# Opening of a two-layer feed-forward kernel: main channels rounded first, and three small steps given to GpSimd

## The reference, cut to what matters

```python
# x: 2 x 4096 x 192, weight: 8 heads x 7 taps
w = softmax(weight, axis=-1)                  # exp(w - max) / (sum + 1e-9)
out[b, s, h, :] = sum_k w[h, k] * x_pad[b, s + k, h, :]   # causal mix of 7 tokens
x = out.reshape(8192, 192)
h = x @ w_in_1                                # 192 x 2048
x = (h * sigmoid(h)) @ w_out_1                # 2048 x 192
h = x @ w_in_2
g = where(h > 0, h, exp(min(h, 0)) - 1)
return g @ w_out_2                            # 8192 x 192, float32
```

## Time and profile before

| what | value |
|---|---|
| runs | 1066.47 to 1066.49 us, median 1066.49 |
| the profiled execution | 1067.03 us |
| its span, first to last instruction | 1065.3 us |
| TensorE busy | 1060.8 us (100%) |
| VectorE, ScalarE, GpSimd busy | 772.0, 638.9, 15.5 us |
| granted TensorE clock, mean | 1.00 |
| chain that ended last | TensorE 100% |

### The profile page before, as it was taken

The page is one execution under the profiler, slowest core; times in us unless marked ns, Lnnn a source line. Parts: engine busy times, 40 slices in busy tenths (PEclk is TensorE's granted clock), DMA queues, the critical chain, the costliest instruction groups (busy, mean ns, idle before and its releaser), DMA issues.

```text
span 1065.3 us, 22927 instructions
## 1 busy us (share of the span) xinstructions
PE 1060.8 (100%) x9728; PEld 1054.7 (99%) x9728; DVE 772.0 (72%) x932; ACT 638.9 (60%) x753; POOL 15.5 (1%) x23
## 2 busy tenths in 40 slices
PE   9999999999999999999999999999999999999998
PEld 8999999999999999999999999999999999999998
DVE  7866679888856647988876654898887664488777
ACT  8767765545566756454666566645465666564544
POOL 2300000000000000000000000000000000000000
PEclk9999999999999999999999999999999999999999
DMA  6510100001000000000110000000011000000001
GB/s 195 104 33 16 54 1 1 17 16 31 16 17 16 17 1 2 11 6 16 31 31 1 17 17 1 1 16 11 7 31 31 2 1 1 1 1 17 12 5 31
DMA packets 19571, 22.28 MB, mean 21 GB/s; under 512 B 3088, under 2 KB 14352, under 8 KB 19472
## 3 DMA queue, kind: packets, MB, share of 16 engines
q1 hardware_dynamic: 16992, 19.64, 6.5%
q0 software_dynamic: 2176, 0.79, 0.7%
q10 hardware_dynamic: 304, 0.40, 0.1%
HBM read 14.52 MB, written 6.29 MB: 20 GB/s over the span
## 4 chain that ended last, share of the span: by engine, by line
PE 100%; ACT 0%; issue 0%; DVE 0%
PE acc L867 51%; PE hid L847 47%; PE acc L998 1%; PE acc L1005 0%; PE acc L976 0%; PE acc L847 0%; PE acc L964 0%; PE acc L967 0%; PE acc L966 0%; ACT stg L442 0%; DVE zero L541 0%
## 5 line engine op out<-in xcount | busy, mean ns | idle before, releaser
L847 PE MATMUL hid<-x,wi 64*128 64x512 f32 x4335 | 658.9, 376 | 0.0
L847 PEld LDWEIGHTS hid<-x,wi 64*128 64x128 f32 x4335 | 545.8, 186 | 1.4 <-DVE wi L591 0.4
L867 PE MATMUL acc<-ghi,wo 64*128 64x512 f32 x3036 | 518.0, 376 | 0.0
L867 PE MATMUL acc<-glo,wo 64*128 64x512 f32 x2024 | 409.1, 376 | 0.0
L867 PEld LDWEIGHTS acc<-ghi,wo 64*128 64x128 f32 x3036 | 406.3, 186 | 0.7 <-issue 0.4
L660 DVE TENSOR_TENSOR glo<-g,ghi 128x1024 fp32r<-128x1024 f32 x214 | 261.3, 1221 | 188.8 <-ACT g L508 136.7
L508 ACT ACTIVATE g<-hid 128x1024 f32<-128x1024 f32 x213 | 217.3, 1020 | 163.8 <-PE hid L847 163.8
L867 PEld LDWEIGHTS acc<-glo,wo 64*128 64x128 f32 x2024 | 292.1, 186 | 0.6 <-DVE glo L649 0.4
L492 ACT ACTIVATE ghi<-hid 128x1024 fp32r<-128x1024 f32 x125 | 128.0, 1024 | 168.2 <-PE hid L847 168.1
L668 DVE SCALAR_TENSOR_TENSOR g<-hid,g 128x1024 f32<-128x1024 f32 x87 | 106.6, 1225 | 3.0
L666 DVE TENSOR_SCALAR g<-g 128x1024 f32<-128x1024 f32 x87 | 60.4, 694 | 60.6 <-ACT g L508 60.4
(11 more groups left out here) (90 smaller groups left out, 370.3 us busy)
## 6 DMA issues: line engine op xcount, KB each, us to landing
stg<-w_in SPq DMA_DIRECT2D x16, 256.0 KB, 3.4
outT<-stg SPq DMA_DIRECT2D x16, 256.0 KB, 2.0
xa<-x_rows SPq DMA_DIRECT2D x15, 259.0 KB, 3.1
stg<-w_out SPq DMA_DIRECT2D x16, 192.0 KB, 4.1
outT<-tail SPq DMA_DIRECT2D x16, 128.0 KB, 2.3
xb<-x_rows SPq DMA_DIRECT2D x30, 65.5 KB, 2.9
wo<-w_out POOLq DMA_DIRECT2D x4, 128.0 KB, 4.8
xa<-x_rows ACTq DMA_DIRECT2D x1, 259.0 KB, 3.0
```

Of the source, the lines that this page charges most:

```text
L847: return eng.matmul(hidden_part(u, t), wt, in_turn(mv), start=t == home and n == 0, stop=t == home and n == 4 if u < LAG else t != home an ...
L867: return eng.matmul(acc[s % 2][:, bank, :], wt[rows, 2 * j + t, cols], in_turn(mv), start=leads and j == 0 and n == 0, stop=not leads and ...
```

## The change

GpSimd gets three steps at the head of its list: it makes part 0 of the rounded last channels of chunk 0, rounds the output weights of piece 0, and makes the two low rests of piece 2, which leaves VectorE's list. ScalarE rounds the main channels ahead of its copy of `mix0`, makes parts 1 to 3 alone after a wait for part 0, and no longer rounds the output weights of piece 0. Waits are added so that counting semaphores stay in order.

```diff
-    APART = (4, 5, 6, 7)
+    APART = (2, 4, 5, 6, 7)
...
@@ gpsimd @@
+            eng.wait_ge(s_tap, 4)
+            eng.wait_ge(s_tapb, NTAP)
+            eng.tensor_scalar(rest_hi(0, 0, LOW)[:, 0:HT], mixb[LOW, :], tstat[LOW, 5:6], None, ALU.mult)\
+               .then_inc(s_chib, 1)
+            eng.wait_ge(s_chib, 1)
+            eng.wait_ge(s_stgo[0], 16)
+            eng.tensor_copy(wo[0][:, 0:2, 0:D], stg_out(0)).then_inc(s_woh, 1)
+            eng.wait_ge(s_woh, 1)
+            eng.wait_ge(s_xlo, 3)
+            low_in_rest(2)
             low_in_rest(4)
...
@@ scalar, hi_out @@
                 eng.wait_ge(s_stgo[q % NSTG], 16 * (q // NSTG + 1))
+                if q == 1:
+                    eng.wait_ge(s_woh, 1)
                 eng.activation(wt[:, :, 0:D], stg_out(q), ACT.Copy).then_inc(s_woh, 1)
...
@@ scalar @@
             hi_in(0)
             hi_in(1)
+            eng.wait_ge(s_tap, 4)
+            conv_hi_a(0)
             eng.wait_ge(s_mix0, 1)
             eng.activation(mixb[:, :], mix0, ACT.Copy).then_inc(s_tapb, NTAP)
-            eng.wait_ge(s_tap, 4)
-            conv_hi_a(0)
             hi_in(2)
-            for part in range(4):
+
+            eng.wait_ge(s_chib, 1)
+            for part in range(1, 4):
                 conv_hi_b(0, part)
             eng.wait_ge(s_tab, 2)
             eng.activation(tstat[:, 6:7], tstat[:, 7:8], ACT.Silu).then_inc(s_tab, 1)
-            hi_out(0)
...
@@ vector @@
             low_in_rest(0)
             low_in_main(2)
-            for q in range(1, 3):
-                low_in_rest(q)
+            low_in_rest(1)
             low_out(0)
```

## The result

The changed kernel takes 1067.91 us (median of 20 runs, 1067.72 to 1068.45), the kernel before 1066.49 (20 runs, 1066.45 to 1066.94): ratio 1.0013, 95% interval 1.0007 to 1.0019. It is 1.42 us slower. That is clear of the interval, though less than the 0.2% which I called the least that counts, and it lies outside my range (1066.2 to 1067.0).

The account below looks back on a forecast made before the run. TensorE, 100% busy, was taken as the bound, with ScalarE setting its waits at 26.5 and 30.7 us. Start 0.00, main channels 0.00, first gate -0.06, late low weights 0.00 gave -0.06: 1066.43 us by the median, range 1066.2 to 1067.0.

Parts of the forecast that it names:

- The start: First real matmul stays at 10.60 us, set by the array's own 0.31 us switch from full to half height; gain 0.00.
- second rival: ScalarE, not the array, sets TensorE's real start: about 10.50, 0.10 us more gained, 1066.3 us; 8%.
- Step 1: ScalarE rounds main channels before copying mixb: worth nothing, since the array is ready later; mixb's copy ends 10.12 instead of 9.84.
- Step 2: GpSimd makes part 0 of the last channels in 0.45 us (0.29 to 0.90), working from 10.61 to about 10.96; hidden.
- the sign that the forecast fails: The forecast fails as a whole if a one-input operation of GpSimd takes over 1 us.
- Step 3: ScalarE makes three parts of the last channels instead of four, ending at 12.60 us; TensorE needs all four at 13.07.
- The first rival: GpSimd is late and TensorE stalls at 13.07 us: up to +1.26 less 0.06, 1067.7 us; 32%.
- TensorE's pair of 13.07: The matmul pair at 13.07 us that needs all four parts of the last channels; forecast to start without a gap.
- Step 4: GpSimd rounds one piece of output weights in 0.6 us; saves 0.06 on ScalarE, leaves 0.03 us to spare at TensorE.
- Step 5: GpSimd makes piece 2's low rests by 14.3 us; first gate's wait shrinks up to 0.2, taken back at 26.5.
- From page to median: Forecast 1066.97 us against the profiled 1067.03, then 1066.43 for the median, that execution being 0.54 above it.

Follow-up runs that it names:

- f4_before_one_more: The kernel before with VectorE's memset of the zeros cut in two, so every later VectorE instruction stands one place further on; 1067.05 us.
- e1_part0_scalar: The changed kernel, but ScalarE makes part 0 again; GpSimd keeps the output-weight rounding and the low rests of piece 2; 1067.05 us.
- h2_weights_alone: The kernel before with only GpSimd rounding the output weights of piece 0; 1066.68 us.
- e2_part0_alone: The kernel before with part 0 alone given to GpSimd, ScalarE waiting for it; 1066.59 us.
- g3_changed_two_more: The changed kernel with VectorE's memset of the zeros cut in three and nothing else; 1067.60 us.

## Why the prediction was wrong

**The start**: the gap between full-height and half-height matmuls was read rightly, the time at which it falls wrongly. The last warm-up matmul starts at 9.62 + 0.82 - 0.38 = 10.06 and the first half-height one at 10.37, 0.31 again:

```profile
9.62 0.82 PE L1013 MATMUL acc<-zero 128*128 128x512 f32 x3
10.37 0.48 PE L862 MATMUL hid<-x,wi 64*128 64x512 f32 x2
```

But 10.60 was that of one execution. In others the warm-up ends earlier, and then the main channels (VectorE's share of them ends at 9.93 to 9.98) set the start, as in the traces that start at 10.03 to 10.08. This is the second rival's mechanism, at 8%, though not its time. Step 1, which gave the new order nothing and a delay of 0.28 for mixb without a price, was wrong for them: TensorE then asks for the last channels 0.5 earlier too, and the new order costs 0.27 alone and 0.78 together with part 0.

**Step 2, part 0, is the step that failed first**, in both its terms. The price was taken from an operation without an operand in memory to scale by, and my upper end from a two-input one: 0.45, at most 0.90. It measured 0.92 free of all company, about 0.72 of it once it has its turn, and 1.69 in its place, over the 1 us that I had named as the sign that the forecast fails. By the best-case figure of the Trainium skill (GPSIMD Engine Reference, on performance against the Vector engine) the estimate was 0.38, less than half; for the plain rounding of 384 elements, 0.50 measured, the estimate of 0.58 by that page is not exceeded. And the turn: I gave it to GpSimd by order of arrival, from one meeting where VectorE's next operation came 0.6 us later. Here L592 came 0.23 later and went first, 0.75 more.

**Step 3** (the fourth part at 12.60) fell with it: 13.58. **The first rival** was the right mechanism, at the right place: TensorE's pair of 13.07, due at 12.85 after the earlier start, came at 13.69, 0.84 late, and 0.10 for the restart. I gave it 32% and up to 1.26 us; its measured 0.95 lies within.

**Step 4**: the rounding at 0.50 for 0.6 was sized well. Its 0.06 on ScalarE didn't show: L518 starts at 15.29, 0.2 after ScalarE's last idle began, for it waits for TensorE as said.

**Step 5**: the first gate's wait shrank by 0.21, as forecast. That what lies behind 26 us would only shift with ScalarE was wrong. I read two turns of GpSimd and VectorE, and passed over the idle of 0.41 "issue" in VectorE's row at 26.08, which decides who goes first. Taking two instructions from VectorE's list removed it. That is 0.50 at unit 5, and f4_before_one_more makes 0.33 there out of nothing else.

**The sum by parts**: order +0.27, part 0 +0.10, rests +0.42, weights +0.19 make 0.98 of the 1.42 (each alone within the noise). Where the remaining 0.44 belong is only argued: order and part 0 together are the likely pair, since giving up either returns about 0.8, but no run has those two alone. Nor do the parts add up elsewhere: order, rests and weights make 0.88 singly and 0.56 together (e1_part0_scalar).

**From page to median**: the profiled execution of the kernel before was 0.54 above the median. The likely reason is that it starts late, not that it was profiled; no trace of an early one of this kernel exists to show it. The profiled executions of part 0 alone and of h2_weights_alone start at 10.04 and 10.08, and took 1066.36 and 1066.46, each the lowest of its kernel.

## What to carry to other kernels

Before a step goes to another engine, measure it there, alone and in its place: a scaled copy of 256 elements with a scalar per partition cost GpSimd 0.92 us, where a plain one of 384 cost 0.50, and beside VectorE 0.75 more. A reordering that seems free is not so when the step behind it has just been given to a slower engine. And where two engines take turns, an idle of 0.4 us of one is part of the schedule: this kernel, tuned to 0.1 us, lost 0.5 by its median to one more instruction in a list, so a change should be compared also with the list padded to its old length.

## What was not expected of the hardware

- VectorE's 64th instruction (waits counted) started 0.36 to 0.41 us late with everything there that it waits for, in all eight traces where the low weights of piece 5 stand at that place, and they start at once in the seven where they stand at another and no wait was added. A start 0.40 us behind a wait that had been met stands at its 1088th instruction in the kernel before, at its 832nd in the changed one and at its 448th in f4_before_one_more, all multiples of 64. All its other starts behind a wait, some 300 a trace between 5 and 1060 us, come within 0.05 us. At most multiples of 64 no idle shows, often because VectorE is still busy there. What happens at these places no run shows; a fetch of instructions was not tried.
- The warm-up's pace changes at a different moment in each trace. In the kernel before three matmuls of 512 columns from 4.15 us take 1.49 (one each 0.43 us), and from 9.85 three take 0.82 (one each 0.22), which is one column a cycle at 1.2 and at 2.4 GHz. Over the sixteen traces the first matmul at the faster pace starts between 3.7 and 7.2 us, while the column of the granted clock says 1.00 throughout. The mix of 14 matmuls took 3.93 us there, 3.71 in the changed kernel and 3.19 in e2_part0_alone:

```profile
4.15 1.49 PE L998 MATMUL acc<-zero 128*128 128x512 f32 x3
5.43 3.93 PE L1005 MATMUL acc<-xb,g 128*128 128x256 f32 x14
```

```profile
5.26 3.19 PE L1011 MATMUL acc<-xb,g 128*128 128x256 f32 x14
...
10.04 0.48 PE L853 MATMUL hid<-x,wi 64*128 64x512 f32 x2 [0.28 <-ACT x L407]
```

With it the real start moves between 10.03 and 10.77 over the traces of this study. How much of that reaches the time depends on the kernel: in g3_changed_two_more, where TensorE waits for the fourth part until 13.70 however early it starts, ten of eleven runs lie within 0.03 us.
- A second thing that moves is a DMA. The low output weights that GpSimd issues (L373 before) between 26.9 and 28.7 us land 4.8 to 5.1 us later in seven of the sixteen traces and 5.8 to 6.3 us later in the other nine, and which edits a kernel has doesn't say which. TensorE's wait for them near 34 us is nothing in eight of the traces and up to 0.5 in the rest, 0.31 of it in the profiled execution of the changed kernel.
